# Attention, mixture of experts and feed-forward in one kernel: one more pair of steps shares its down products, and the third phase's input blocks are made in two steps

## What is computed

```python
def _attn_ref(q, k, v):                       # 2 x 8 heads, 768 positions, 64 wide
    ...
    a = a / (np.sum(a, axis=-1, keepdims=True) + 1e-09)
    return np.matmul(a, v_all)                # 32-key window and 24 block summaries

def _moe_ref(x, domain_probs, w1, w2):        # 1536 tokens, 512 wide, 4 experts of 1024
    p = domain_probs / (domain_probs.sum(-1, keepdims=True) + 1e-09)
    for e in range(E):
        h = np.maximum(x @ w1[e], 0.0)
        out += p[:, e:e + 1] * (h @ w2[e])

def _moe2_ref(x, w_in, w_out):                # 512 -> 2048 -> 512
    h = x @ w_in
    g = h * (1.0 / (1.0 + np.exp(-1.702 * h)))
    return g @ w_out
```

## Time and profile before

| | us |
|---|---|
| median of three runs | 817.17 |
| profiled execution | 818.92 |
| its span, first to last instruction | 817.1 |
| TensorE busy | 795.5 (97%) |
| GpSimd busy | 581.9 (71%) |
| VectorE busy | 561.8 (69%) |
| ScalarE busy | 426.4 (52%) |
| mean granted TensorE clock | 0.991 of full speed |

### The profile page before, as it was taken

The page is one execution under the profiler, slowest core; times in us unless marked ns, Lnnn a source line. Parts: engine busy times, 40 slices in busy tenths (PEclk is TensorE's granted clock), DMA queues, the critical chain, the costliest instruction groups (busy, mean ns, idle before and its releaser), DMA issues.

```text
span 817.1 us, 14162 instructions
## 1 busy us (share of the span) xinstructions
PE 795.5 (97%) x4894; PEld 780.5 (96%) x4894; DVE 561.8 (69%) x1197; ACT 426.4 (52%) x941; POOL 581.9 (71%) x405
## 2 busy tenths in 40 slices
PE   5889999999999999999999999999999999999997
PEld 4779999999999999999999999999999999999996
DVE  6989656666665566677777778666666665678686
ACT  3865454454445454546555554434555553656662
POOL 3688755656665699688798794776588783598793
PEclk8989999999999999999999999999999999999999
DMA  9949656385444354446354443444544544373512
GB/s 275 282 120 323 258 199 209 142 285 210 149 189 162 142 224 153 172 165 226 110 211 165 166 156 143 149 187 158 216 178 158 204 161 191 119 281 142 181 52 78
DMA packets 39958, 148.93 MB, mean 182 GB/s; under 512 B 16208, under 2 KB 17360, under 8 KB 36688
## 3 DMA queue, kind: packets, MB, share of 16 engines
q1 hardware_dynamic: 39888, 148.03, 50.0%
HBM read 100.81 MB, written 47.21 MB: 181 GB/s over the span
## 4 chain that ended last, share of the span: by engine, by line
PE 89%; DVE 5%; issue 2%; POOL 1%; ACT 1%; DMA 1%; SPq 0%; DVEq 0%; ACTq 0%; POOLq 0%
PE bank L1705 29%; PE bank L1707 28%; PE bank L1706 28%; PE bank L1660 2%; PE bank L1697 1%; PE bank L1671 1%; DVE bank L1468 1%; DMA v_cols<-v_t 1%; DVE masked L1330 1%; DVE row_sum_e L1340 1%; DVE v_sum L1318 0%; POOL xb_last_lo L779 0%; ACT prob L974 0%; POOL prob L711 0%; ACT sig L1059 0%
## 5 line engine op out<-in xcount | busy, mean ns | idle before, releaser
L1398 DVE TENSOR_TENSOR xa<-bank,xa 128x384 f32<-128x384 f32 x208 | 115.9, 557 | 136.7 <-PE bank L1707 133.9
L1705 PE MATMUL bank<-h_hi,wd_hi 128*128 128x384 f32 x448 | 150.2, 335 | 0.0
L1707 PE MATMUL bank<-h_lo,wd_hi 128*128 128x384 f32 x448 | 149.9, 335 | 0.0
L1706 PE MATMUL bank<-h_hi,wd_lo 128*128 128x384 f32 x448 | 149.8, 334 | 0.0
L1065 ACT ACTIVATE h_hi<-bank 128x384 fp32r<-128x384 f32 x112 | 55.0, 491 | 134.1 <-DVE bank L1463 110.8
L755 POOL TENSOR_TENSOR wd_lo<-stage,wd_hi 128x1024 fp32r<-128x1024 f32 x27 | 65.1, 2413 | 81.7 <-ACT wd_hi L1022 81.5
L1705 PE MATMUL bank<-xb_other_hi,wu_hi 128*128 128x384 f32 x336 | 112.6, 335 | 0.2 <-ACT snap L1049 0.2
L822 POOL TENSOR_TENSOR wd_lo<-stage,wd_hi 128x512 fp32r<-128x512 f32 x60 | 89.5, 1497 | 32.4 <-ACT wd_hi L1121 32.3
L1707 PE MATMUL bank<-xb_other_lo,wu_hi 128*128 128x384 f32 x336 | 112.4, 335 | 0.0
L1706 PE MATMUL bank<-xb_other_hi,wu_lo 128*128 128x384 f32 x336 | 112.4, 334 | 0.0
L1049 ACT ACTIVATE snap<-bank 128x384 f32<-128x384 f32 x141 | 69.0, 489 | 72.0 <-PE bank L1707 71.1
(11 more groups left out here) (123 smaller groups left out, 2068.5 us busy)
## 6 DMA issues: line engine op xcount, KB each, us to landing
stage<-weights SPq DMA_DIRECT2D x25, 1024.0 KB, 4.9
split<-wu_hi SPq DMA_DIRECT2D x24, 896.0 KB, 3.6
split<-wu_lo SPq DMA_DIRECT2D x24, 896.0 KB, 5.4
wu_hi<-split SPq DMA_DIRECT2D x23, 896.0 KB, 6.3
wu_lo<-split SPq DMA_DIRECT2D x23, 896.0 KB, 8.0
stage<-weights SPq DMA_DIRECT2D x23, 512.0 KB, 4.4
k_win<-k_w SPq DMA_DIRECT2D x8, 720.0 KB, 8.2
v_win<-v_w SPq DMA_DIRECT2D x8, 576.0 KB, 8.9
```

The source lines that it names most:

```text
L1398: nc.vector.tensor_tensor(at, y_bank(g, t), at, ALU.add).then_inc(y_taken, 1)
L1705: nc.tensor.matmul(dst, w_h, a_h, start=first, stop=False, skip_group_check=True)
L1706: nc.tensor.matmul(dst, w_l, a_h, start=False, stop=False, skip_group_check=True)
L1707: return nc.tensor.matmul(dst, w_h, a_l, start=False, stop=last, skip_group_check=True)
```

## The change

- Steps 28 and 29 become a pair (`PAIRED` ends at 30 in place of 28). The places of the down weights are turned by one from step 30 on (`wd_place`, `held_2`).
- Phase 2 is prepared in steps 30 and 31 instead of 29 to 31 (`AHEAD`). GpSimd makes the low parts of blocks 0, 2 and 1; VectorE those of 3 and 6 in step 31 and of 4 and 5 in step 32, the first step that reads them (`low_by_dve`, `low_ready`).
- ScalarE may overwrite a block's buffer as soon as the last pair product that reads it is done (`high_moved`). In steps 30 to 32 ScalarE takes the raw weights of the next step behind snap 2, not ahead of the first hidden tile.
- In the feed-forward half, VectorE takes pair product P4 ahead of the last gate; the first pair's P1 and P5 wait for the takes of their own bank only; in the last step snap 2 stands ahead of a held block.

```diff
-AHEAD = (None, 3, 3, 6)
+AHEAD = (None, 3, 2, 6)
-PAIRED = ((MOE_STEPS, 28), (FFN0 + PAIRS_2, STEPS))
+PAIRED = ((MOE_STEPS, 30), (FFN0 + PAIRS_2, STEPS))
...
+        def low_by_dve(ph, i):
+            return ph == 0 or ph == 2 and MADE_2.index(i) >= BY_POOL_2
...
+        def wd_place(g):
+            return (g + (g >= PAIRED[0][1])) % NWD
...
@@ GpSimd's loop
+                if (ph, part) == (2, 1):
+                    low_moved(ph, 1)
+                    low_down(g)
+                    sum_moved(ph, 3)
                 if more:
                     sum_weights(g + 1)
...
                     sum_moved(ph, 1)
+                    low_moved(ph, 0)
                     low_down(g)
-                    low_moved(ph, 0)
                     low_moved(ph, 2)
                     sum_moved(ph, 2)
-                    low_moved(ph, 1)
-                    low_down(g + 1)
                     continue
                 if ph == 2 and part == 1:
-                    low_moved(ph, 3)
-                    sum_moved(ph, 3)
                     sum_moved(ph, 4)
-                    low_moved(ph, 6)
+                    low_sums(g + 1)
                     low_down(g + 1)
-                    low_moved(ph, 4)
-                    low_moved(ph, 5)
                     continue
@@ ScalarE
                 if ph == 2:
-                    act.wait_ge(y_done, takes(PAIRED[0][1]))
+                    name = next(n for n in ORDER if MOVED[n] == i)
+                    act.wait_ge(y_done, summed(PAIRED[0][1] - 2, name, 1))
...
-                    high_held(g - 1, "P6")
+                    if g + 1 < STEPS:
+                        high_held(g - 1, "P6")
                     keep(g, 1)
+                    if g + 1 == STEPS:
+                        high_held(g - 1, "P6")
...
                     keep(g, 1)
                 if more:
+                    if g == FFN0 or ph == 2:
+                        high_raw(g + 1)
                     high_sums(g + 1)
@@ VectorE's loop
                     add_c12(g)
+                    if g >= FFN0:
+                        take_product(g - 2, "P4", 0)
                     gate(g, "C12")
-                    take_product(g - 2, "P4", 0)
+                    if g < FFN0:
+                        take_product(g - 2, "P4", 0)
...
                     take_y(g - 1, 3)
+                    if preparing(g) == (2, 1):
+                        low_moved(3, 2)
+                    if g == FFN0:
+                        low_moved(4, 2)
...
                 take_y(g - 1, 4)
+                if g == FFN0:
+                    low_moved(5, 2)
                 add_c22(g)
...
                 gate(g, "C12")
+                if preparing(g) == (2, 1):
+                    low_moved(6, 2)
@@ TensorE, pair_product
                 if name in ("P1", "P5"):
-                    pe.wait_ge(y_taken, taken(g - 2, {"P1": "P4", "P5": "P3"}[name], d) if paired(g - 1) else takes(g))
+                    pe.wait_ge(y_taken, taken(g - 2, {"P1": "P4", "P5": "P3"}[name], d) if paired(g - 1) else
+                               takes(g) - KT + {"P1": 0, "P5": 2}[name] + d + 1)
```

More of the change, by code:

```diff
@@ L481, in held_2 @@
             at = slice(DM * (n % 2), DM * (n % 2 + 1))
-            return wd_hi[:, n // 2, at], wd_lo[:, n // 2, at]
+            place = (n // 2 + (g >= PAIRED[0][1])) % NWD
+            return wd_hi[:, place, at], wd_lo[:, place, at]
         def held_source(name):
@@ L1214, in _ @@
                 else:
-                    if more:
-                        high_raw(g + 1)
-                    if ph == 2:
-                        if part == 0:
-                            high_down(g, 0)
-                            high_down(g, 1)
-                            high_moved(ph, 0)
-                        elif part == 1:
-                            high_moved(ph, 3)
+                    if (ph, part) == (2, 1):
+                        high_down(g, 0)
+                        high_down(g, 1)
+                        high_moved(ph, 3)
+                    if g == FFN0:
+                        high_moved(2, 5)
+                    elif more and ph != 2:
+                        high_raw(g + 1)
                     if ffn:
@@ L1785, in down @@
                     w = slice(DM * f + P * d, DM * f + P * (d + 1))
-                    last = three(y_bank(g, t), wd_hi[:, g % NWD, w], wd_lo[:, g % NWD, w],
+                    last = three(y_bank(g, t), wd_hi[:, wd_place(g), w], wd_lo[:, wd_place(g), w],
                                  h_hi[:, g % 2, 2 * f + c, :], h_lo[:, g % 2, 2 * f + c, :], f == 0, f == 1)
```

60 lines of the change are left out of this document (33 added, 27 removed).

## The result

The kernel after takes **825.77 us** (median of 4 runs, 824.47 to 826.63) against 817.22 (4 runs, 815.74 to 817.66): a ratio of 1.0092, 95% interval 1.007 to 1.0115. The forecast was 824.4 us, with a range of 819.3 to 827.8. The profiled execution of after took 825.16 us with a span of 822.8, where that of before had 818.92 and 817.1.

A forecast was written before the change was run, and what follows sets the result against it. TensorE's matmuls plus the holes between them were taken as the bound. Terms -2.08 - 0.49 + 5.0 + 2.3 + 2.1 + 1.1 + 0.3 - 1.02 give +7.2 us; forecast 824.4 us, range 819.3 to 827.8.

The forecast's parts named there:

- The pair: Steps 28 and 29: 16 down products become 14 pair products, no hole expected; -2.08 us.
- The hole of step 31: TensorE waits ahead of P4 for snap 3, queued behind step 32's weights; +5.0 us, bounds 4.3 and 5.5.
- The meeting with VectorE's block 3: Step 31: block 3's subtraction beside GpSimd's sum 3 pushes GpSimd's next operation by some 0.7 us.
- The half clock: Behind the hole of step 31 the clock drops to half; +2.3 us, bounds nothing and 3.4.
- P7's hole: Step 32: P7 waits for block 4, made behind VectorE's fourth take; 1.7 to 2.9 us, taken as 2.1.
- P4's hole: Step 32: P4 waits for block 5, made behind VectorE's fifth take; 0.65 to 1.8 us, taken as 1.1.
- The rival that priced each meeting so: Every meeting of VectorE and GpSimd on the port pair costs a whole operation: 826.4 us or a little more; chance 0.07.
- The load order is mostly covered: Store of step 32's weights ahead of step 33's load: up to 1 us in step 32's copy, mostly covered by P4's hole.
- The feed-forward half: Waits mended in steps 43, 45 and 47; sum -1.02 us, bounds 0 and -1.5.
- 43 and 45: Steps where VectorE's take of P4 comes before the gate and is in time; -0.36 us twice.
- 41: Step where the take is no longer waited for but a ScalarE and GpSimd chain loses it again; 0, bound -0.4 us.
- Step 47: Its P7 waits for a snap that moves ahead of a held block; -0.30 us.

The follow-up runs named there:

- x1: The kernel after with ScalarE's snap 3 of step 31 ahead of the weights of step 32; 823.14 us, ratio 1.0075.
- x7: The kernel after with snap 3 of step 31 between the raw weights and the sum weights; 821.73 us, one run.
- x8: The kernel after with snap 3 of step 31 between the sum weights and block 6; 825.49 us, one run.
- x6: The kernel after with the load of step 33's weights issued ahead of the store of step 32's; 825.36 us, ratio 1.0115.
- x3: The kernel after with the edit of x1 and that of x2 together; 824.1 us, ratio 1.0101.
- x9: x3 with the load of step 33's weights issued ahead of the store of step 32's; 816.44 us, ratio 0.9987.
- x11: x10 without the three edits of the feed-forward half; 816.61 us, ratio 0.9974.
- x5: The kernel after with x8's snap 3, x2's blocks, x6's load, and GpSimd's additions for step 32 earlier in its queue; 817.04 us, ratio 0.9983.
- x2: The kernel after with VectorE's low parts of blocks 4 and 5 earlier in its queue in step 32; 822.51 us, ratio 1.0061.
- x10: x5 with block 6 made in step 32 behind the fourth take, and snap 3 of step 32 ahead of step 33's weights; 814.76 us, ratio 0.9964.

## Why the prediction was right, and where it was off

**The pair** gave 2.13 us, as forecast: step 29 lasts 11.44 us with 11 products and no hole.

**The hole of step 31.** The count along GpSimd's queue, from the low part of the down weights to the first addition, was 10.50 us and came out at 10.49. The meeting with VectorE's block 3 did what was forecast: the first addition lasts 1.45 us, not 0.74 (+0.71), and snap 3 ends 16.33 us into the step. The counted 15.7 + 0.7 was 16.4. x1 shows that the hole hangs on snap's place: with the copy ahead of the weights, at 550.77, P4 of step 31 starts in its turn.

**The half clock** lost 2.18 us of a forecast 2.3. The step "of 5.0 us nearly half is lost" came near for this hole, but no row of before sized it, so that is luck, and as a rule it is wrong. x7 loses 1.52 of 2.74 us and x8 1.59 of 4.13: the loss is not a share of the hole.

**Step 32.** P7's hole, 1.76 us, lies at the lower end of 1.7 to 2.9: the block was hardly met there (1.03 us). That it came out below the 2.1 taken is luck of the meeting, not of the count. P4's hole is the term that was mis-sized, 1.1 against 2.30 us, and beyond its upper bound of 1.8. The counted step was "subtraction 2.76 to 3.71 behind P7's start, up to 1.8 with a meeting". The bound took the meeting from a row where the two overlapped in part (2.13 us); here they start together and VectorE stands for nearly all of GpSimd's operation (2.62 us). That is the rule of the Trainium skill (SBUF — State Buffer, "Who interferes with whom"), that the second fully blocks until the first is done; this trace agrees, with 1.67 us of waiting beside an operation of 1.81. The rival that priced each meeting so gave 826.4 us, and the median, 825.77, lies between it and the forecast. It was too high on P7, though, since what decides is how much of the other operation is left. One sum fits both rows: VectorE's 0.95 us, and what is left of GpSimd's operation when VectorE starts, less 0.13 (719.52 - 718.21 = 1.31 gives 2.13; 578.71 - 576.91 = 1.80 gives 2.62). The rows before allowed it, but the start of GpSimd's operation would have had to be counted too, and that hung on the late load: with the load early, in x6, 1.93 us of subtraction and a hole of 1.62 were left.

**"The load order is mostly covered"** was true, and it was the least examined sentence. For the kernel after it cost nothing to be seen in the time (x6), and 0.7 us in the hole ahead of P4. With the two other faults gone it cost 7.7 us (x3 against x9). The forecast of the change could afford that; the forecasts of x1 and x3 could not, and missed by 3.2 and 8.0 us.

**The feed-forward half.** 43 and 45 gave 0.36 us each and 41 nothing, as forecast. Step 47 was mis-sized: -0.30 forecast, +0.03 measured. Its hole ahead of P7 is gone, but P5's second product now takes 1.43 us, released by VectorE's `xb_first_lo`; in x11, without the mends, that product takes 1.10 and P7 1.15 again, behind a hole of 0.24. The forecast had looked for the next late one behind the mend in step 41, and not in step 47. Which of the edits makes P5 late was not tried apart.

**The range** held the result, 1.4 us above the forecast. On TensorE's ledger 0.8 of this is there: P4's hole (+1.2) and step 47 (+0.3), less P7's hole (-0.3) and small shares of the other terms (-0.4 in all). So errors of both signs met in the sum, and that it came out within 0.8 us is in part luck. The other 0.6 us, between the ledger and the two medians, no run explains.

## What to carry to other kernels

When an in-order queue has a short copy that TensorE needs standing behind work that waits for another engine, look for the same pattern one step on: a hole covers the waits behind it, and an edit that removes it pays only when the next reader's inputs are in time too. Price an edit against the hole that covers it, and try cures together as well as one by one: here a single exchange of a load and a store was worth nothing alone and 7.7 us with two others. Where VectorE takes work over from GpSimd, put it where GpSimd is not in a long operation with two operands in SBUF, or count what is left of that operation when VectorE starts, up to the whole of it.

## What the runs showed of the hardware

*Holes and the clock.* TensorE ran matmuls without a pause right ahead of and behind each of these holes. Some stand close to another one: that of 2.30 us in after comes 3.1 us of matmuls behind that of 1.76.

| hole us | kernel | clock behind it | lost us |
|---|---|---|---|
| 1.45, 1.54, 1.62, 1.68, 1.68, 1.68, 1.76 | x5, x8, x6, x6, x1, x7, after | stays at full | 0 |
| 2.30 | after | stays at full | 0 |
| 2.24 | x8 | half | 1.67 |
| 2.74 | x7 | half | 1.52 |
| 3.81 | x1 | half | 1.44 |
| 4.13 | x8 | half | 1.59 |
| 4.83 | x2 | half | 2.13 |
| 4.86 | after | half | 2.18 |
| 4.86 | x6 | half | 2.73 |
| 4.94 | x3 | half | 2.04 |

I had not expected that 2.24 us halves it in one run and 2.30 does not in another, nor that equal holes of 4.86 us lose 2.18 and 2.73. Each is one profiled execution. The clock is told by the granted clock and the products: 1.04 us each at full (2.4 GHz), 1.92 at half (1.2 GHz), apart from some 0.1 us more in the first product behind any wait.

*A load behind two stores.* In x3 the two loads of 1024 KB took a median of 8.8 us from issue to landing with two stores of 896 KB issued just ahead on the same queue; over the whole kernel the median of such a load is 4.9. By an estimate from these two medians, about 3.8 of the 6.62 us that GpSimd waits in x3 are the slower landing, the rest the later issue; no run parts the two.

*A meeting can be total.* VectorE's subtraction of 128x768 took 0.95, 1.03, 1.09, 1.34, 2.27, 2.54 and 2.62 us. What it took beyond 0.95 follows, to 0.02 us, what was left of the GpSimd operation that had started first, less 0.13: 0.21 left gives 1.03 (after, 572.97), 0.52 gives 1.34 (x10), 1.45 gives 2.27 (after, 550.32), 1.72 gives 2.54 (x5), 1.80 gives 2.62. The engine that comes second pays: in x6 the two start at 572.98 and 572.99, VectorE takes its 0.95 us and GpSimd's low part of 1024 columns 3.21 instead of 2.40. GpSimd's addition of 128x256 takes 0.74 us or, just behind a VectorE subtraction that waited, 1.45.
